# One kernel, three stages: keys of attention tiled 128+128+128+64, and attention run apart from the first GEMM

## The reference, cut to what matters

```python
scores = scale * np.matmul(q, k.transpose(0, 1, 3, 2))   # (2, 12, 448, 448)
scores = cap * np.tanh(scores / cap)
attn = np.exp(scores - max); attn = attn / (attn.sum(-1) + 1e-09)
x = np.matmul(attn, v)                       # -> (896, 768) after joining heads
h = x @ w_in; x = np.maximum(0.01 * h, h) @ w_out         # 768 -> 2048 -> 768
x = rms_norm(x) * rms_g
out = (silu(x @ w_gate) * (x @ w_val)) @ w_out2           # 768 -> 1536 -> 768
```

## Time and profile before

| | |
|---|---|
| runs shown, median | 647.5 us (645.27 to 647.73, 3 runs) |
| the profiled execution | 645.47 us, span 643.7 us |
| mean granted clock | 0.989 |
| PE busy | 623.4 us, 97% |
| DVE busy | 274.2 us, 43% |
| POOL busy | 219.6 us, 34% |
| ACT busy | 153.8 us, 24% |

### The profile page before, as it was taken

How to read it: one execution, slowest core, us unless ns; L and a number is a source line. 1 busy time by engine, 2 the same in 40 slices (tenths; PEclk the granted TensorE clock), 3 DMA queues, 4 the chain that set the end, 5 groups by cost and what they waited for, 6 DMA issues and landing times.

```text
span 643.7 us, 7531 instructions
## 1 busy us (share of the span) xinstructions
PE 623.4 (97%) x3024; PEld 530.0 (82%) x3024; DVE 274.2 (43%) x403; ACT 153.8 (24%) x195; POOL 219.6 (34%) x138
## 2 busy tenths in 40 slices
PE   5999989999979999999999999999999999999998
PEld 3444556666779998999999999999999999999998
DVE  3254535563479999233312335534444354210000
ACT  5767625544101111011110123111111112000000
POOL 1000212443364545243423443535454453323000
PEclk9999979999979999999999999999999999999999
DMA  6224342322233334212201121312122210023101
GB/s 192 57 73 115 76 108 65 107 72 71 64 113 105 116 99 124 89 34 66 63 37 57 50 61 38 97 52 74 50 74 73 75 52 23 24 74 123 38 24 38
DMA packets 32930, 47.37 MB, mean 74 GB/s; under 512 B 17792, under 2 KB 21120, under 8 KB 32896
## 3 DMA queue, kind: packets, MB, share of 16 engines
q1 hardware_dynamic: 32896, 46.89, 24.3%
HBM read 44.04 MB, written 2.80 MB: 73 GB/s over the span
## 4 chain that ended last, share of the span: by engine, by line
PE 94%; DVE 3%; POOL 1%; DMA 1%; ACT 1%; issue 1%; SPq 0%; DVEq 0%
PE ps L724 27%; PE ps L704 18%; PE ps L651 18%; PE ps L767 13%; PE ps L635 12%; PE ps L621 5%; DVE x_raw L451 1%; DMA qk_raw<-in_qk 1%; DVE g_hi L490 0%; POOL act_lo L330 0%; POOL w_lo L297 0%; DMA sums<-x_raw 0%; POOL v2a_lo L336 0%; ACT probs L363 0%; PE ps L734 0%
## 5 line engine op out<-in xcount | busy, mean ns | idle before, releaser
L297 POOL TENSOR_TENSOR w_lo<-w_raw,w_hi 128x768 fp32r<-128x768 f32 (+1 forms) x68 | 133.8, 1968 | 263.5 <-DVE w_hi L481 263.5
L481 DVE CAST w_hi<-w_raw 128x768 fp32r<-128x768 f32 (+1 forms) x68 | 39.5, 582 | 179.2 <-issue 98.1
L651 PE MATMUL ps<-x_hi,w_hi 128*128 128x448 f32 x192 | 81.0, 422 | 6.3 <-POOL w_lo L297 3.5
L635 PE MATMUL ps<-probs,v_ones 112*128 112x448 f32 x192 | 81.5, 553 | 3.3 <-DVE x_raw L451 2.9
L724 PE MATMUL ps<-x_hi,w_hi 128*128 128x448 f32 x288 | 81.9, 366 | 0.0
L724 PE MATMUL ps<-x_hi,w_lo 128*128 128x448 f32 x288 | 81.8, 365 | 0.0
L724 PE MATMUL ps<-x_lo,w_hi 128*128 128x448 f32 x288 | 81.8, 365 | 0.0
L651 PE MATMUL ps<-x_lo,w_hi 128*128 128x448 f32 x192 | 71.8, 374 | 0.0
L651 PE MATMUL ps<-x_hi,w_lo 128*128 128x448 f32 x192 | 71.6, 373 | 0.0
L635 PEld LDWEIGHTS ps<-probs,v_ones 112*128 112x128 f32 x192 | 34.7, 190 | 32.8 <-issue 31.2
L724 PEld LDWEIGHTS ps<-x_lo,w_hi 128*128 128x128 f32 x288 | 54.1, 188 | 4.3
(11 more groups left out here) (77 smaller groups left out, 845.3 us busy)
## 6 DMA issues: line engine op xcount, KB each, us to landing
w_raw<-in_w_in SPq DMA_DIRECT2D x32, 384.0 KB, 3.2
w_raw<-in_w_out SPq DMA_DIRECT2D x12, 512.0 KB, 3.6
qk_raw<-in_qk SPq DMA_DIRECT2D x12, 448.0 KB, 3.8
w_raw<-in_w_gate SPq DMA_DIRECT2D x12, 384.0 KB, 3.0
w_raw<-in_w_val SPq DMA_DIRECT2D x12, 384.0 KB, 2.9
v_raw<-in_w_out SPq DMA_DIRECT2D x12, 384.0 KB, 3.0
v_ones<-in_v SPq DMA_DIRECT2D x24, 112.0 KB, 2.8
recip_row<-recips SPq DMA_DIRECT2D x24, 112.0 KB, 2.8
```

What stands on the lines that cost most here:

```text
L297: pool.tensor_tensor(w_lo[u % 2][:, 0:n], w_raw[u % 2][:, 0:n], w_hi[u % 2][:, 0:n].bitcast(F32), ALU.subtract).then_inc(w_lo_done, 1)
L481: dve.tensor_copy(w_hi[u % 2][:, 0:n], w_raw[u % 2][:, 0:n]).then_inc(w_hi_done, 1)
L635: last = pe.matmul(ps[:, PV + h, 0:S], v_ones[p % 2][R, c:c + 2 * D], probs_of(p, t, h), start=(t == 0), stop=(t == T - 1))
L651: last = pe.matmul(ps[:, HP + u % 2, 0:S], w[u % 2][:, c * 128:(c + 1) * 128], x[:, (b * KD + c) * S:(b * KD + c + 1) * S], start=(c == 0 ...
```

## The change

Keys are tiled 128 + 128 + 128 and a rest of 64, T = 4 still counting the score tiles of a pair. In the three main tiles each head has its own matmuls. For the rest the host lays out k as a block diagonal (the other head's rows are zero), so one matmul on all 128 partitions gives head 0's 64 keys on output partitions 0 to 63 and head 1's on 64 to 127. A pair has 7 score and probability tiles of 448 columns where it had 8. q and k have 960 columns where they had 896. v comes in four DMAs a pair in place of two, and the ones of v_ones are set over the whole buffer first, so that the first two loads of v wait for that. Score tiles use three pairs of banks (0 to 5) in turn, PV banks 6 and 7, and the first GEMM banks 4 and 5. TensorE's list is: all four score tiles of pair p, all of PV of pair p-1; and when all pairs are done, the 32 units. Nothing is interleaved. The lists of SP and VectorE change with it: the turn p of both now serves pair p, not p-1, and lo parts of all units' results are made by VectorE.

```diff
-        SC, PV, HP = 0, 4, 6
+        PV, HP = 6, 4
...
+        def bank_of(p, i):
+            return 2 * ((T * p + i) % 3)
...
                 at_least(sp, pv_done, p - 1)
+                if p < 2:
+                    sp.wait_ge(v_ones_set, p + 1)
                 for h in range(2):
-                    dst = tiles(v_ones[p % 2][R, cols(h, T * 2 * D)], 2 * D)[:, :, HEAD[h]]
-                    sp.dma_start(dst, v[p, h]).then_inc(v_in[p % 2], 16)
+                    dst = tiles(v_ones[p % 2][:, h * MAIN * 128:(h + 1) * MAIN * 128], 128)[:, :, HEAD[h]]
+                    sp.dma_start(dst, v[p, :, h * MAIN:(h + 1) * MAIN]).then_inc(v_in[p % 2], 16)
+                    sp.dma_start(v_ones[p % 2][HEAD[h], 2 * MAIN * 128 + h * D:2 * MAIN * 128 + (h + 1) * D],
+                                 v[p, HEAD[h], 2 * MAIN]).then_inc(v_in[p % 2], 16)
...
-            for p in range(PAIRS + 1):
+            for p in range(PAIRS):
                 if p + 2 < PAIRS:
                     load_qk(p + 2)
                 if p + 1 < PAIRS:
                     load_v(p + 1)
-                for u in units_of(p)[0:1]:
-                    load_w(w_in[u + 2], u + 2, KD * 128)
-                if p > 0:
-                    spread_sums(p - 1)
-                    store_recip(p - 1)
-                    load_recip_row(p - 1)
-                for u in units_of(p)[1:2]:
-                    load_w(w_in[u + 2], u + 2, KD * 128)
-            for u in range(OVERLAPPED + 2, U_OUT):
+                spread_sums(p)
+                store_recip(p)
+                load_recip_row(p)
+            for u in range(2, U_OUT):
                 load_w(w_in[u % N1], u, KD * 128)
...
             split_qk(0)
-            for p in range(PAIRS + 2):
-                if p + 1 < PAIRS:
-                    split_qk(p + 1)
-                if p == FIRST - 1:
+            split_qk(1)
+            for p in range(PAIRS):
+                if p + 2 < PAIRS:
+                    split_qk(p + 2)
+                keep_x(p)
+                if p == 2:
                     weight_hi(0, KD * 128)
                     weight_hi(1, KD * 128)
-                if 0 < p <= PAIRS:
-                    keep_x(p - 1)
-                if p > 1:
-                    normalise(p - 2)
-                if 0 < p <= PAIRS:
-                    reciprocal(p - 1)
...
+                if p > 0:
+                    normalise(p - 1)
+                reciprocal(p)
+            for u in range(N1):
                 weight_hi(u + 2, KD * 128)
-                leaky_all(u)
+                leaky(u)
+                if u == 1:
+                    normalise(PAIRS - 1)
...
-                at_least(pe, tanh_done, 4 * p + t - 1)
+                at_least(pe, tanh_done, T * p + i - 2)
...
                 for k, q in ((hi, hi), (hi, lo), (lo, hi)):
+                    if i < MAIN:
+                        for h in range(2):
+                            last = pe.matmul(ps[:, bank + h, 0:S], k[HEAD[h], k_c], q[HEAD[h], 0:S],
+                                             start=(k is hi and q is hi), stop=(k is lo))
+                    else:
+
+                        last = pe.matmul(ps[:, bank, 0:S], k[:, k_c], q[:, 0:S],
                                          start=(k is hi and q is hi), stop=(k is lo))
                 last.then_inc(scores_done, 1)
...
+            def weigh(p):
+
+                pe.wait_ge(exp_done, 2 * p + 1)
+                pe.wait_ge(v_in[p % 2], 64 * (p // 2 + 1))
+                at_least(pe, x_raw_done, p)
+                for t in range(MAIN):
+                    if t == 2:
+                        pe.wait_ge(exp_done, 2 * p + 2)
+                    for h in range(2):
+                        c = (h * MAIN + t) * 128
+                        pe.matmul(ps[:, PV + h, 0:S], v_ones[p % 2][:, c:c + 128],
+                                  probs[p % 2][:, (2 * t + h) * S:(2 * t + h + 1) * S], start=(t == 0), stop=False)
+                c = 2 * MAIN * 128
                 for h in range(2):
+                    last = pe.matmul(ps[:, PV + h, 0:S], v_ones[p % 2][HEAD[h], c:c + 128],
+                                     probs[p % 2][HEAD[h], 2 * MAIN * S:(2 * MAIN + 1) * S], start=False, stop=True)
+                last.then_inc(pv_done, 1)
...
+            for p in range(PAIRS + 1):
                 if p < PAIRS:
+                    for i in range(T):
+                        scores(p, i)
                 if p > 0:
+                    weigh(p - 1)
+            for u in range(U_OUT):
+                unit_in(u)
```

More of the change, by code:

```diff
@@ L18, in build @@
 def build(nc, qk, v, cap, w_in, w_out, w_gate, w_val, w_out2, rms_g, out, recips):
-    PAIRS, _, S2 = qk.shape
-    S = S2 // 2
+    PAIRS, _, QK = qk.shape
+    S = out.shape[0] // 2
     B, D, T = 2, 64, 4
     ROWS = S // T
+    MAIN = S // 128
+    REST = S - MAIN * 128
     NP = PAIRS // B
@@ L31, in build @@
     SAFE = 80.0
-    assert NP == KD and ROWS == 112 and N1 == 16 and S == 448
+    assert NP == KD and ROWS == 112 and N1 == 16 and S == 448 and REST == D and QK == S + MAIN * 128 + 2 * REST
     U_OUT = 2 * N1
     U_GV = U_OUT + 2 * KD
-    FIRST = NP + 1
-    OVERLAPPED = 12
     with ExitStack() as ctx:
@@ L73, in build @@
         place["at"] = G1
[L74 to L78, removed]
+        qk_raw = [buf(f"qk_raw{s}", QK, F32) for s in range(2)]
+        qk_hi = [buf(f"qk_hi{s}", QK, F32R) for s in range(2)]
+        qk_lo = [buf(f"qk_lo{s}", QK, F32R) for s in range(2)]
+        v_ones = [buf(f"v_ones{s}", (2 * MAIN + 1) * 128, F32) for s in range(2)]
+        probs = [buf(f"probs{s}", (2 * MAIN + 1) * S, F32) for s in range(2)]
         x_raw = [buf(f"x_raw{s}", 2 * S, F32) for s in range(2)]
@@ L183, in tiles, with probs_of @@
             return t.rearrange("p (t c) -> p t c", c=n)
[L185 to L191, removed]
+        def bank_of(p, i):
+            return 2 * ((T * p + i) % 3)
+        def probs_of(p, i, n):
+            return probs[p % 2][:, 2 * i * S:(2 * i + n) * S]
         @block.sync
@@ L286, in _ @@
             for s in range(2):
-                for h in range(2):
-                    dst = tiles(v_ones[s][R, cols(h, T * 2 * D)], 2 * D)[:, :, HEAD[1 - h]]
-                    pool.memset(dst, 1.0).then_inc(v_ones_set, 1)
+                pool.memset(v_ones[s][:, :], 1.0).then_inc(v_ones_set, 1)
             pool.memset(ident[:, :], 0.0).then_inc(ident_done, 1)
@@ L351, in _, with tanh @@
         def _(act):
-            def tanh(p, t):
-                act.wait_ge(scores_done, 4 * p + t + 1)
+            def tanh(p, i):
+                n = 2 if i < MAIN else 1
+                act.wait_ge(scores_done, T * p + i + 1)
                 at_least(act, pv_done, p - 1)
-                dst = tiles(probs[p % 2][R, 2 * t * S:(2 * t + 2) * S], S)
-                act.activation(dst, ps[R, SC + 2 * (t % 2):SC + 2 * (t % 2) + 2, 0:S],
+                act.activation(tiles(probs_of(p, i, n), S), ps[:, bank_of(p, i):bank_of(p, i) + n, 0:S],
                                ACT.Tanh, scale=scale_reg).then_inc(tanh_done, 1)
             def exp(p, half):
-                act.wait_ge(tanh_done, 4 * p + 2 * half + 2)
-                c = probs[p % 2][R, 4 * half * S:(4 * half + 4) * S]
-                act.activation(c, c, ACT.Exp, scale=cap_reg, bias=capc[R, 6:7]).then_inc(exp_done, 1)
+                act.wait_ge(tanh_done, T * p + 2 * half + 2)
+                c = probs_of(p, 2 * half, 4 - half)
+                act.activation(c, c, ACT.Exp, scale=cap_reg, bias=capc[:, 6:7]).then_inc(exp_done, 1)
             def leak_part(u):
@@ L374, in _ @@
             act.reg_load(scale_reg, capc[0:1, 4:5].bitcast(mybir.dt.int32))
[L376 to L389, removed]
+            for p in range(PAIRS):
+                tanh(p, 0)
+                tanh(p, 1)
+                exp(p, 0)
+                tanh(p, 2)
+                tanh(p, 3)
+                exp(p, 1)
+            for u in range(U_OUT):
                 leak_part(u)
@@ L439, in split_qk @@
                 dve.wait_ge(qk_in[p % 2], 16 * (p // 2 + 1))
-                at_least(dve, scores_done, 4 * (p - 1))
+                at_least(dve, scores_done, T * (p - 1))
                 dve.tensor_copy(qk_hi[p % 2][:, :], qk_raw[p % 2][:, :]).then_inc(qk_hi_done, 1)
@@ L485, in leaky @@
                 dve.wait_ge(leak_done, u + 1)
-                at_least(dve, g_lo_done, u - 1)
-                hi = (g0_hi, g1_hi)[u // N1]
+                hi, lo = ((g0_hi, g0_lo), (g1_hi, g1_lo))[u // N1]
                 dve.tensor_tensor(g_full[u % 2][:, :], ps[:, HP + u % 2, 0:S], leak[u % 2][:, :], ALU.max).then_inc(g_done, 1)
@@ L610, in _, with scores @@
         def _(pe):
-            def scores(p, t):
-                if t == 0:
+            def scores(p, i):
+                if i == 0:
                     pe.wait_ge(qk_lo_done, p + 1)
-                at_least(pe, tanh_done, 4 * p + t - 1)
+                at_least(pe, tanh_done, T * p + i - 2)
```

(40 more changed lines are left out.)

11 lines of the change are left out of this document (removed).

## The result

The kernel after takes 675.8 us (674.95 to 679.13, 4 runs) against 646.9 us before: ratio 1.0459, 95% interval 1.0418 to 1.0501. 670 was forecast, 658 to 688 the range. It is slower by 29 us, where 22 were expected. The profiled execution's span is 673.4 us, its mean granted clock 0.972 (before 0.989).

What follows compares the result with a forecast made beforehand. TensorE bound the kernel before; after, a 12.5 us loop through the qk load would pace attention. Later attention and unit 2, plus slower units, sum to +22.3 us, 645.5 to 667.8; median 2.0 higher gives 670, range 658 to 688.

Steps and rivals of the forecast that it cites:

- The mechanism: Attention: keep_x waits for split_qk, the qk load and the previous pair's row, a once-a-pair loop of 12.5 us.
- Steps of the loop: From keep_x's end: sums 2.47, store issue 0.43, row issue 1.41, qk issue 1.19, landing 4.0, split to 11.35, keep_x 1.11 us.
- The pair: One attention pair takes the loop's 12.5 us (12.1 to 13.3), against 10.12 before and TensorE's own 7.9.
- the 12 to 13 us that were to show it: Sign of being right: keep_x every 12 to 13 us for pairs 1 to 9.
- Start and end: keep_x(0) ends at 23.5, keep_x(11) at 153.6; unit 2 starts at 165.6, 5.8 us late; units end at 274.7.
- the prediction's own range: Nine periods x (-0.4 to +0.8), 64-row PV +1.5 in two pairs, start and end 3 either way: 661 to 683 us.
- TensorE's saving: PV: two 64-row matmuls together take 0.755 us, saving 0.75 us a pair, hidden by the loop except in the last two pairs.
- A sign of being wrong: keep_x every 8 us, or TensorE's waits in attention naming ScalarE or v_ones.
- Rival 1: Attention: the loop doesn't bind, TensorE sets the pace at 7.9 us a pair; about 627 us, chance 0.08.
- Rival 2: Attention: the clock stays low between gaps and sets the pace, 15.3 us a pair; 695 us, chance 0.09.
- Rival 3: Attention: half of the loop is hidden, a pair at 10 to 11 us; 648 to 657 us, chance 0.07.
- The two rules: Skill's DMA estimate: loop 0.75 us a pair shorter, 663 in all; skill's clock rule: kernels restart at the low clock after every wait.

Runs made afterwards that it cites:

- e1: Kernel after the change with the q and k load issued one pair sooner in SP's list, nothing else changed: 644.8 us, ratio 0.999 to the kernel before.
- e10: e6 with v's four loads a pair issued by GpSimd instead of SP: 629.0 us, ratio 0.976 to the kernel before.
- e11: e10 with the old tiles (4 of 112 keys, 8 full PV matmuls): 631.2 us, ratio 0.977 to the kernel before.
- e4: Kernel after the change with the old tiles (4 of 112 keys, two v loads a pair), new order kept: 679.9 us, ratio 1.051 to the kernel before.
- e6: Kernel after the change with q and k loaded one pair ahead, v two pairs ahead, first-GEMM weight loads and casts early: 632.2 us, ratio 0.980 to the kernel before.
- e3: Kernel after the change with two more full PV matmuls a pair (tile 0 done twice): 679.5 us, ratio 1.052 to the kernel before.
- e2: Kernel after the change with keep_x(p) ahead of split_qk(p+2) in VectorE's list, loads left: 674.6 us, ratio 1.043 to the kernel before.
- e9: e2 with 12 small unused matmuls filling TensorE's wait ahead of each pair's scores, from pair 2 on: 666.5 us, ratio 1.032 to the kernel before.
- e12: e10 with the loads of q and k on GpSimd's queue too: 625.1 us, ratio 0.968 to the kernel before.

## Why the prediction was right, point by point

- **The mechanism was right.** keep_x(p) behind split_qk(p+2), behind a load issued after the row of p-1: e1 undoes that order and nothing else, gets 31 us back and takes VectorE's wait for q and k from 70.0 to 0.6 us.
- **Steps of the loop** against the earlier trace rows: sums landed 2.47 us after keep_x's end (forecast 2.47), store to row issue 1.42 (1.41), row to q and k issue 1.19 (1.19), split and hand-over as forecast.
- **The pair was mis-sized:** 13.52 us, not 12.5, 9.2 us over nine turns, and over the 13.3 given as its upper end. Five of the nine turns lie in the 12 to 13 us that were to show it. By the chain: three stores took 2.44, 3.36 and 2.46 us where the others took 1.41, 4.0 us in all; q and k landed after 3.99 to 4.56, together 2.3 over nine times 4.0; turn 2 has the two weight casts and GpSimd's subtraction beside it, sums_eps there 6.3 us behind keep_x in place of 2.5: 3.8. The other steps are 0.9 shorter. The 3.8 was there to be seen: in the kernel before, VectorE's two multiplications at 183.07 take 2.78 us in place of 1.26, beside GpSimd's subtraction at 183.23. The prediction counts 0.5 us for normalise(11) and nothing for turn 2. Turn 2 is at 48.7:
```profile
48.72 1.02 DVE L463 CAST w_hi<-w_raw 128x768 fp32r<-128x768 f32 x2
...
49.35 4.26 POOL L293 TENSOR_TENSOR w_lo<-w_raw,w_hi 128x768 fp32r<-128x768 f32 x2 [46.32 <-DVE w_hi L463]
49.65 4.44 DVE L450 TENSOR_TENSOR x_norm<-x_raw,recip_row 64x448 f32<-64x448 f32 x2
```
- **Start and end:** keep_x(0) ended at 23.35 (23.5). keep_x(9) to keep_x(11) took 16.6 (17.6). keep_x(11) to unit 2: 12.8 (12.0), TensorE idle 6.44 (5.8). Units 2 to 30: 107.8 (109.1). 9.2 - 0.15 - 1.0 + 0.8 - 1.3 = 7.5 us, the whole of the difference between 22.3 and 29.8. The terms of the prediction's own range add up to 663 to 682, not 661 to 683; the measured time lies in either.
- **TensorE's saving** was real and hidden: 0.75 us a pair was taken, e10's good turns are 0.8 us shorter than e11's, and e4's pair equals the kernel's.
- **A sign of being wrong came once:** TensorE waits for v_ones, 2.31 us ahead of the PV at 154.80. That is the last pair, outside the loop; v was priced at nothing, and in the nine turns it did cost nothing.
- **Rival 1** (TensorE sets the pace) is what e10's good turns show at 8.1 us. Moving the load of q and k alone brings a pair to 9.9 us (e1); for turns of 8.1 one after another v's loads had to move too (e6, e10). **Rival 2** (the lower clock) did not set the pace here, since e3's extra work left the pair as it was; in most turns of e2 it is part of the pace. Its price was taken too high, at 5.9 / 2 = 2.95 us: a turn's scores took 4.1 to 5.0 us where the clock was low at first or fell under way, and 2.7 at full clock (117.60 to 120.33), so 1.4 to 2.2 us. **Rival 3** did not occur.
- **The two rules weighed.** The estimate from the Trainium skill's DMA: Bandwidth & Descriptors (Anatomy of one DMA) gave 663; the rows gave 670 and were nearer. Of the lower clock after each wait (the Trainium skill, TensorE: Matmul & The Clock Gate, HAM oscillation) e2 and e9 show the repeated case: 12.9 us a turn against 11.3 with the gap filled. It does not come after every wait, though: three of e2's ten turns kept the full clock.

Open: what makes a 3.5 KB store take 3.4 us instead of 1.4 (in the kernel before up to 2.5), and whether the tiling's full 0.8 us a pair can be had at e12's order, which was run with the new tiles only.

## What to carry to other kernels

Follow a load that was not edited through the new order: ask behind which wait its issue now stands in the queue, and how many turns back that wait reaches. Here going from two turns back to one turned a path with 20 us to run in into a loop of 13. When one such loop is cut, the next one (here v, then the row, then the sums) is close behind, so price all loads of a turn before moving one.

## What the hardware did that I had not expected

In the kernel before, the clock fell inside the gap. In the kernel after it can also fall after the work has begun again. Timeline and stretches (length, busy by engine, clock, DMA) of the kernel after:
```profile
78.17 0.48 PE L593 MATMUL ps<-qk_hi 64*128 64x448 f32 x2 [3.50 <-DVE qk_lo L425]
78.47 0.37 PE L593 MATMUL ps<-qk_lo,qk_hi 64*128 64x448 f32 x2
...
78.88 0.58 PE L593 MATMUL ps<-qk_hi 64*128 64x448 f32 x2
```
```profile
74.70:78.00 3.30, 0.00 (x0) 0.00 (x0) 1.71 (x2) 0.00 (x0) 0.00 (x0) 1.00 0.45 123
78.00:83.00 5.00, 4.83 (x23) 3.83 (x24) 3.64 (x8) 3.64 (x4) 0.00 (x0) 0.66 0.03 3
```
TensorE stands still for 3.50 us at a granted clock of 1.00. The first three steps of scores are 0.2 to 0.3 us apart, and from 78.88 on they are 0.37; the granted clock is 1.00 from 78.0 to 78.5 and 0.50 from 79.0 to 82.0. The price of a gap is then paid by the work after it, even where the clock looks full during the gap.
